# Chunk one's routing logits: 12 narrow fp32 products, or 4 side by side in column groups and 3 that sum them

## The reference, cut to what matters

```python
# dense layer: 1152 tokens, 512 -> 2048 -> 512
h = x @ w_in
g = np.where(h >= 1, h, np.where(h <= -1, 0.0, (h + 1) ** 2 / 4))
x = g @ w_out
# routed layer: 8 experts
logits = x @ w_gate                       # [1152, 512] @ [512, 8]
expert_idx = np.argmax(logits, axis=1)
gate_w = softmax(logits)[arange, expert_idx]
# tokens take places in their expert in order; then relu(disp @ w1[e]) @ w2[e], times gate_w
```

## Time and profile before

| | |
|---|---|
| median of 3 runs | 313.24 us (312.58 to 313.87) |
| the profiled execution | 313.38 us, of which its span is 311.4 us |
| PE busy | 301.4 us, 97% of the span |
| DVE, ACT, POOL busy | 70%, 49%, 44% |
| granted TensorE clock, mean | 0.997 |
| share of PE in the chain that ended last | 91% |

### The profile page before, as it was taken

One profiled execution on the slowest core, in us unless ns is written; L12 is line 12 of the kernel. 1 busy time (PEld: TensorE's weight loads), 2 busy tenths in 40 slices (PEclk: granted clock), 3 DMA queues, 4 the chain that ended last, 5 costly groups with the idle time before them and its releaser, 6 DMA issues.

```text
span 311.4 us, 7140 instructions
## 1 busy us (share of the span) xinstructions
PE 301.4 (97%) x2766; PEld 250.8 (81%) x2766; DVE 217.6 (70%) x573; ACT 153.2 (49%) x337; POOL 136.1 (44%) x152
## 2 busy tenths in 40 slices
PE   7799999999999999999999999999999999999894
PEld 6466676676666988887999999898989899995663
DVE  5799998999978366897884547956774588842200
ACT  1777767757866244655551443446354555202020
POOL 4686997998998300464780003014011333100031
PEclk9999999999999999999999999999999999999998
DMA  8999889951637700000000408660034039079940
GB/s 151 159 201 214 210 155 192 210 134 64 174 78 197 217 3 2 0 2 2 0 2 7 71 0 337 216 95 11 2 49 67 0 105 422 17 278 365 379 146 8
DMA packets 75048, 38.48 MB, mean 124 GB/s; under 512 B 66009, under 2 KB 66017, under 8 KB 73989
## 3 DMA queue, kind: packets, MB, share of 16 engines
q1 hardware_dynamic: 72340, 36.74, 44.9%
q10 hardware_dynamic: 2416, 0.59, 1.1%
q0 software_dynamic: 256, 0.67, 0.7%
HBM read 32.66 MB, written 5.39 MB: 122 GB/s over the span
## 4 chain that ended last, share of the span: by engine, by line
PE 91%; DVE 2%; DMA 2%; SPq 2%; issue 1%; ACT 0%; POOL 0%; POOLq 0%; DVEq 0%
PE bank_a L1829 17%; PE bank_b L1829 17%; PE bank_out L1786 6%; PE bank_b L1889 4%; PE bank_pt L1739 4%; PE bank_pt L1889 4%; PE bank_a L1687 4%; PE bank_a L1763 3%; PE bank_a L2065 2%; PE bank_out L1862 2%; PE bank_b L2065 2%; PE bank_out L1783 2%; PE bank_b L1682 2%; PE bank_out L2202 2%; PE bank_b L2075 2%; PE bank_a L2075 2%
## 5 line engine op out<-in xcount | busy, mean ns | idle before, releaser
L718 POOL TENSOR_SCALAR prob<-prob,rl,gate_loc 128x512 f32<-128x512 f32 (+3 forms) x64 | 41.4, 662 | 13.0 <-DVE rl L1236 13.0
L1829 PE MATMUL bank_a<-x_hi,win_hi 128*128 128x288 f32 x128 | 39.3, 307 | 0.0
L1829 PE MATMUL bank_b<-x_hi,win_hi 128*128 128x288 f32 x128 | 38.1, 297 | 0.0
L1829 PE MATMUL bank_b<-x_lo,win_hi 128*128 128x288 f32 x128 | 38.0, 297 | 0.0
L1829 PE MATMUL bank_b<-x_hi,win_lo 128*128 128x288 f32 x128 | 38.0, 297 | 0.0
L1829 PE MATMUL bank_a<-x_hi,win_lo 128*128 128x288 f32 x128 | 38.0, 297 | 0.0
L1829 PE MATMUL bank_a<-x_lo,win_hi 128*128 128x288 f32 x128 | 38.0, 296 | 0.0
L965 ACT ACTIVATE g_raw<-bank_a,biases 128x576 f32<-128x576 f32 x16 | 11.9, 743 | 51.0 <-DVE sq L1313 51.0
L902 ACT ACTIVATE prob<-prob,negmax 128x512 f32<-128x512 f32 (+3 forms) x64 | 35.0, 550 | 1.2 <-DVE negmax L1186 1.2
L747 POOL TENSOR_TENSOR x_lo<-xT,x_hi 128x1152 fp32r<-128x1152 f32 x4 | 10.6, 2661 | 49.7 <-ACT x_hi L915 49.7
L802 POOL TENSOR_TENSOR w_lo<-w_sb,w_hi 128x512 fp32r<-128x512 f32 x8 | 11.3, 1415 | 48.2 <-ACT w_hi L1008 48.2
(11 more groups left out here) (329 smaller groups left out, 796.3 us busy)
## 6 DMA issues: line engine op xcount, KB each, us to landing
w_sb<-in_moe_w_dram SPq DMA_DIRECT2D x6, 2048.0 KB, 11.0
win_raw<-in_moe_w_in_dram SPq DMA_DIRECT2D x4, 1024.0 KB, 5.5
wout<-in_moe_w_out_dram SPq DMA_DIRECT2D x4, 1024.0 KB, 5.9
win_raw<-in_moe_w_in_dram SPq DMA_DIRECT2D x1, 4096.0 KB, 13.3
out_dram<-zero_row SPq DMA_DIRECT2D x8, 288.0 KB
x_d<-x_rows SPq DMA_DIRECT2D x32, 72.0 KB, 2.1
v_sb<-in_v_dram SPq DMA_DIRECT2D x16, 128.0 KB, 2.6
qn<-in_q_dram SPq DMA_DIRECT2D x24, 72.0 KB, 5.5
```

The lines of the kernel that those rows point to most:

```text
L718: pool.tensor_scalar(prob[u][:, h, :], prob[u][:, h, :], rl[:, c:c + 1], gate_loc[:, 2 * j + h:2 * j + h + 1], ALU.mult, ALU.mult).then_in ...
L1829: last = pe.matmul(h_bank(d)[:, t, :], w[:, m, f:f + P], x[c % 2][:, m, :], start=(m == 0 and n == 0), stop=(m == KT - 1 and n == 2))
```

## The change

- `wg_pad` [128, 4, 32] is new: the gate weights of each feature tile m, filled up from 8 to 32 columns with zeros. POOL makes it behind `few_iota` in one memset and one copy.
- `first_logits` moves up by one hidden step on PE, from behind hidden(1, 3) to behind hidden(1, 2). It now makes 4 products side by side, one for each m, each into its own 32 rows of `bank_t`, with 32 columns of `wg_pad` as weights and all 288 columns of `x2T[:, m, :]` as moving data. It waits for `s_ye` as before, and in addition for `s_pad` (POOL) and `s_wpe` (the last reader of `bank_t`).
- DVE copies `bank_t` to `lgT` behind add_terms(1, 1), ahead of clip(1, 3).
- `token_logits`, so far for c > 1 alone, is called for c = 1 too, behind hidden(1, 3), and waits for that copy (`s_xle`).
- `logits(c, 0)` waits for `s_xle` in the place of `s_wpe`, since `bank_t` is now read by that copy.

```diff
@@ -186,6 +186,7 @@
         hot = [sb(f"hot{n}", [ST, NR, P], BF16, at=(wg_rep_at, zero_at)[n // 2] + 2 * NR * P * (n % 2))[0] for n in range(NCH)]
+        wg_pad, _, _ = sb("wg_pad", [P, KT, 32], F32, at=zero_at)
...
@@ -820,6 +824,10 @@
             pool.iota(few_iota[:, :], [[0, GROUPS], [1, FEW]], base=0, channel_multiplier=0,
                       allow_small_or_imprecise_dtypes=True).then_inc(s_fio, 1)
+            pool.memset(wg_pad[:, :, :], 0.0).then_inc(s_pad, 1)
+            pool.wait_ge(s_pad, 1)
+            pool.wait_ge(s_wg, 16 * 5)
+            pool.tensor_copy(wg_pad[:, :, 0:E], wg[:, :, :]).then_inc(s_pad, 1)
             x_lo_part(2)
@@ -1508,6 +1516,9 @@
                     if d > 0:
                         add_terms(c, d - 1)
+                    if c == 1 and d == 2:
+                        dve.wait_ge(s_xl1, 1)
+                        dve.tensor_copy(lgT[:, :], bank_t[:, 0:CHUNK]).then_inc(s_xle, 1)
                     if c > 0 and d == 7:
@@ -1855,7 +1866,7 @@
                 if q == 0:
-                    pe.wait_ge(s_wpe, 1)
+                    pe.wait_ge(s_xle, 1)
@@ -1898,15 +1909,18 @@
             def first_logits():
 
                 pe.wait_ge(s_ye, KT)
-                for r in range(NR):
-                    for m in range(KT):
-                        last = pe.matmul(bank_o[0:ST, LG_AT + r * E:LG_AT + (r + 1) * E], x2T[:, m, r * ST:(r + 1) * ST], wg[:, m, :],
-                                         start=(m == 0), stop=(m == KT - 1))
-                last.then_inc(s_lg, 1)
+                pe.wait_ge(s_pad, 2)
+                pe.wait_ge(s_wpe, 1)
+                for m in range(KT):
+                    last = pe.matmul(bank_t[32 * m:32 * m + 32, 0:CHUNK], wg_pad[:, m, :], x2T[:, m, :], start=True, stop=True)
+                last.then_inc(s_xl1, 1)
 
             def token_logits(c):
 
-                pe.wait_ge(s_lte, c - 1)
+                if c == 1:
+                    pe.wait_ge(s_xle, 1)
+                else:
+                    pe.wait_ge(s_lte, c - 1)
                 pe.wait_ge(s_sel, 1)
@@ -2011,9 +2025,9 @@
-                    if c == 1 and d == 3:
+                    if c == 1 and d == 2:
                         first_logits()
-                    if c > 1 and d == 3:
+                    if c > 0 and d == 3:
                         token_logits(c)
```

More of the change, by code:

```diff
@@ L380, in build_program @@
         s_fio = sem("s_fio")
+        s_pad = sem("s_pad")
+        s_xl1 = sem("s_xl1")
+        s_xle = sem("s_xle")
         s_list = sem("s_list")
```

## The result

| | before | changed |
|---|---|---|
| median of 6 runs each | 312.97 us (312.33 to 313.87) | 311.58 us (310.92 to 311.94) |
| ratio | | 0.9949, 95% interval 0.9925 to 0.9974 |
| the profiled execution | 313.38 us, span 311.4 us | 311.82 us, span 309.9 us |

The changed kernel is faster by 0.5%, some 1.6 us by the ratio. 312.5 us had been forecast, 0.7 us less than before, so the direction is right and the gain about twice the forecast. In a later comparison of 12 runs with 35 of the kernel before, the ratio was 0.9962 (0.9944 to 0.9979), 1.2 us.

What follows compares the result with a forecast made beforehand. PE, busy without a gap from the edit on, was taken as the bound: −2.07 us removed, +0.81 and +0.56 us added, −0.70 us in all. From the 313.24 us median that gave 312.5 us, range 311.5 to 313.6.

Steps and rivals of the forecast that it cites:

- What bounds the kernel: From the edit to 283.9 us PE never waits, so time taken from its queue moves everything behind it equally.
- The sum: PE's time at the edit: −2.07 + 0.81 + 0.56 = −0.70 us, with ends −0.89 and −0.18.
- The one rule that spoke against the change: Some 60 cycles per matmul: 24 old records would cost 0.6 us, and the change would lose 0.8 us.
- The waits: New waits at the edit cost nothing: copy slack some 1.9 us, `s_ye` nearly 6 us, `wg_pad` over 8 us.
- that cover: DVE's copy lies in 1.80 us of idle time; without it, PE's wait would be paid microsecond for microsecond.
- B: Rival: PE's wait for the DVE copy before the summing products eats the gain; ceiling 0.7 us, 313.4 us; chance 0.03.
- C: Rival: the four products run in turn, 3.25 us, total +1.7 us, 315.1 us; chance 0.01.
- D: Rival: the change works but no time is seen, PE's gain only −0.18 us, 313.2 us; chance 0.10.
- A: Rival: PE's 1.17 us stop at 291.58 vanishes (311.5 us) or a second comes (313.85 us); chance 0.07 each.
- A's lower half: The 1.17 us stop at 291.58 falls under a wait of the last batch: 311.5 us; chance 0.07.
- Within 0.5%: Whole kernel: the change stays within 0.5%, 1.57 us, of no change; chance 0.91.

Runs made afterwards that it cites:

- three others of the twelve: Changed kernel with the four products and DVE copy one hidden step later, twelve runs: 313.49 us, ratio 1.0019; four had low mean clocks and took 314.0 to 314.8 us.
- the three comparisons: Changed against before: 0.9949 at first, 0.9962 in 12 runs against 35, and, with the second weight transfer issued later in both kernels, 0.9979 less 1.0026.
- The lean pair: PE waits that an earlier PE wait already covers left out: of the changed kernel 311.08 us, ratio 0.9943; of the kernel before 312.69 us, ratio 0.9941.

## Why the prediction was right and wrong

*What bounds the kernel.* Right. PE was never idle from the edit to 283 us in either kernel, and A to B moved by what was taken from PE's queue.

*The sum.* Right: −0.73 us by the insertions and −0.76 us over the whole stretch, for −0.70 forecast. The four products cost 0.81 us as taken, the three 0.53 for 0.56, the twelve 2.07 before. The lone call of the earlier trace rows was the right row; half of the double call, 0.65, would have been too low. The one rule that spoke against the change, that of the Trainium skill (TensorEngine Tiling (Array Packing), section Instruction Overhead) of some 60 cycles for each matmul, whether of 1 column or of 60, holds here in its second half only. 8 and 32 moving columns do cost the same, but 0.083 us a record, and not the 0.025 us worked out from it.

*The waits.* Right, with a slack of two microseconds for the copy. "If that cover were gone, the price would be PE's wait, microsecond for microsecond" does not hold for every execution: in the profiled one the wait of 1.26 us brought a lower clock with it, for 1.5 us more, and three others of the twelve have a low mean clock too.

*The rivals* (the prediction's letters, not the four starts above). B, C and D didn't occur. C leaned on the Trainium skill's rule (TensorE: Matmul & The Clock Gate, section Part 3, The mechanism) that weight loads overlap with running products only where the row group differs. That is a rule on the loads, and by itself it would not put the products in turn; 0.81 us for the eight records, of 0.41 us each, shows that they ran side by side. A is where the prediction failed. It named the stop at 291.58 and said that its place may hang on the position in the stream, which is so. But it says "The change alters the number of PE's instructions ahead of it by a few" and "the shift is small", and never counts. The count is 18, and 18 instructions there are 8 records and a transpose, 3.63 + 0.24 − 3.41 = 0.46 us of work that PE does ahead of the stop in place of behind it. As the block's time is set by the weights and not by this place, the stop shrinks by as much. The step that failed is this term, put at nothing: it is −0.46 us by the durations, −0.47 us by the way from the end of the stop to C in six executions. With it the forecast is −0.70 − 0.46 = −1.2 us, and the three comparisons gave −1.6, −1.2 and −1.5 us. The measured median, 311.58, lies just inside the range, 311.5 to 313.6, near what A's lower half gives, 311.5. That is luck: there the stop was to vanish under a wait, and it only shrank. "Within 0.5%" with 0.91 was too sure for a sum that left out a term of two thirds of its size.

*What is left.* Between −1.2 and the −1.6 us of the first comparison lies scatter that no run here takes apart: the stop has 0.66 or 1.21 us in the same kernel, C to D 11.86 or 11.95 us, and the way to A takes 167.4 to 168.0 us with and without the change. The lean pair, which shows no local gain between its two ratios, stays open as well.

## What to carry to other kernels

Where one engine is busy without a gap, a local sum from the distances of starts is good to some hundredths of a microsecond, so the rest of a surprise is to be sought where that engine does stand still. A stop without a releaser in the midst of equal instructions is a candidate for a late block of instructions, above all where narrow products use instructions up fast while large transfers run: count the instructions that an edit adds or takes ahead of it, waits included, and put the work that they move past the stop into the sum. Waits that an earlier wait covers cost nothing where the engine is busy, but leaving out 48 instructions of them moved the stop away here and gave the fastest version, 0.9943 (0.9940 with the loads split). Where it can be had, keep large transfers out of the microseconds in which such a block is due.

## What the runs showed of the hardware

- A block of PE's instructions is one packet of 16 KB. It moved 0.2 us ahead of B with idle DMA engines, and 2.2 to 3.1 us behind it among weights in the ten executions with a stop ahead of C. There PE went on 2.2 to 2.5 us after it started to move.
- The stop stands behind 5058 instructions of PE's stream in eleven executions of nine kernels; smaller gaps stand 256 behind that in two executions and 512 behind it in three.
- Pauses of PE of 1.26 us in the dense stretch and of 1.90 and 4.99 us in the last batch were followed by a granted clock of 0.54, 0.56 and 0.50 for some 3 us; pauses of 1.33, 1.34 and 1.48 us in the last batch were not (1.00).
- fp32 products with 96 columns of weights cost 0.083 us a record with 8 and with 32 moving columns.
